# Routing between MLP and experts: order of TensorE's products, the expert list, loads and fetches at the transition

## The reference

```python
def _moe2_ref(x, w_gate, w1, w2):          # x 3072 x 512, 8 experts, w1 512 x 1024, w2 1024 x 512
    logits = x @ w_gate
    expert_idx = np.argmax(logits, axis=1)
    logits_shift = logits - logits.max(-1, keepdims=True)
    probs = np.exp(logits_shift)
    probs /= probs.sum(-1, keepdims=True) + 1e-09
    gate_w = probs[np.arange(N), expert_idx]
    for e in range(E):
        mask = expert_idx == e
        xe = x[mask]
        h = np.maximum(xe @ w1[e], 0.0)
        ye = h @ w2[e]
        out[mask] = gate_w[mask, None] * ye
```

## Time and profile before

| | us |
|---|---|
| median of 3 runs (lowest, highest) | 1026.34 (1026.3, 1027.01) |
| profiled execution | 1028.64 |
| its span | 1027.0 |
| PE busy | 999.0 (97%) |
| PEld busy | 818.5 (80%) |
| DVE busy | 647.8 (63%) |
| ACT busy | 583.8 (57%) |
| POOL busy | 403.4 (39%) |

### The profile page before, as it was taken

The page is one execution under the profiler, slowest core; times in us unless marked ns, Lnnn a source line. Parts: engine busy times, 40 slices in busy tenths (PEclk is TensorE's granted clock), DMA queues, the critical chain, the costliest instruction groups (busy, mean ns, idle before and its releaser), DMA issues.

```text
span 1027.0 us, 19832 instructions
## 1 busy us (share of the span) xinstructions
PE 999.0 (97%) x6222; PEld 818.5 (80%) x6223; DVE 647.8 (63%) x1211; ACT 583.8 (57%) x1255; POOL 403.4 (39%) x393
## 2 busy tenths in 40 slices
PE   7988999999999999999999999998999999999998
PEld 5766778888888888888888888886788888888886
DVE  5877788878876886787778788855224424225221
ACT  7877778766776676677666776724124324225221
POOL 3676354444544554455445546621111111112111
PEclk9999999999999999999999999989999999999999
DMA  8999613940890194059001202119112412411111
GB/s 308 347 410 353 261 42 114 363 140 12 273 347 28 62 359 153 4 188 300 0 10 41 103 21 73 42 44 350 69 41 67 174 50 83 152 41 41 32 51 36
DMA packets 58272, 143.26 MB, mean 139 GB/s; under 512 B 4711, under 2 KB 10471, under 8 KB 58224
## 3 DMA queue, kind: packets, MB, share of 16 engines
q1 hardware_dynamic: 51424, 121.07, 33.3%
q0 software_dynamic: 6800, 21.56, 6.2%
HBM read 71.08 MB, written 72.32 MB: 140 GB/s over the span
## 4 chain that ended last, share of the span: by engine, by line
PE 88%; ACT 3%; DMA 3%; DVE 2%; issue 2%; SPq 1%; POOL 0%; POOLq 0%; ACTq 0%; DVEq 0%
PE PS L667 25%; PE PS L509 25%; PE PS L540 14%; PE PS L549 14%; ACT prob L815 2%; PE PS L533 2%; PE PS L687 2%; PE PS L611 1%; PE PS L526 1%; DVE PS L997 1%; DMA out<-y_sb,idx_s 1%; DMA qk<-qk_all 1%; PE PS L707 1%; PE PS L581 1%; DMA pad_rows<-rows_by_expert 1%
## 5 line engine op out<-in xcount | busy, mean ns | idle before, releaser
L509 PE MATMUL PS<-xs,weights 128*128 (+1 forms) x1152 | 282.7, 394 | 0.0
L509 PEld LDWEIGHTS PS<-xs,weights 128*128 128x128 f32 x1152 | 212.7, 188 | 43.1
L667 PE MATMUL PS<-weights,g_hi 128*128 128x512 f32 x768 | 238.0, 391 | 1.3 <-POOL g_lo L1342 0.8
L1342 POOL TENSOR_TENSOR g_lo<-g_sb,g_hi 128x512 fp32r<-128x512 f32 x96 | 124.3, 1295 | 275.2 <-ACT g_hi L895 275.2
L667 PEld LDWEIGHTS PS<-weights,g_hi 128*128 128x128 f32 x768 | 143.0, 188 | 35.0 <-issue 2.9
L667 PE MATMUL PS<-weights,g_lo 128*128 128x512 f32 x384 | 149.6, 390 | 0.0
L876 ACT ACTIVATE b_ln<-PS,cf 128x512 f32<-128x512 f32 x96 | 66.0, 687 | 141.6 <-PE PS L509 141.6
L540 PE MATMUL PS<-weights,xg_hi 128*128 (+1 forms) x448 | 143.0, 401 | 0.5 <-issue 0.5
L549 PE MATMUL PS<-weights,h_hi 128*128 (+1 forms) x432 | 135.8, 395 | 1.3 <-issue 1.3
L1345 POOL TENSOR_TENSOR den<-den,b_r 128x512 f32<-128x512 f32 x96 | 128.9, 1343 | 2.1 <-ACT b_r L903 2.1
L1046 DVE TENSOR_TENSOR xg_lo<-PS,xg_hi 128x512 fp32r<-128x512 f32 x29 | 20.0, 690 | 127.3 <-ACT xg_hi L840 127.3
(11 more groups left out here) (189 smaller groups left out, 1584.7 us busy)
## 6 DMA issues: line engine op xcount, KB each, us to landing
rows_by_expert<-pad_rows SPq DMA_DIRECT2D x16, 1799.0 KB, 20.4
e_raw<-w_exp SPq DMA_DIRECT2D x34, 512.0 KB, 6.5
qk<-qk_all SPq DMA_DIRECT2D x32, 480.0 KB, 7.0
rows_by_expert<-pad_rows SPq DMA_DIRECT2D x8, 1542.0 KB, 20.0
vw<-v_all SPq DMA_DIRECT2D x32, 384.0 KB, 6.7
rows_by_expert<-pad_rows SPq DMA_DIRECT2D x8, 1285.0 KB, 17.7
w_raw<-w_mlp SPq DMA_DIRECT2D x16, 512.0 KB, 8.5
pad_rows<-rows_by_expert POOLq DMA_DIRECT2D x30, 257.0 KB, 3.0
```

The costliest lines, as they stand in the source:

```text
L509: last = pe.matmul(PS[:, H_BANK + f % 2, :], w[:, wp], rhs, start=k == 0, stop=k == 3 * KT - 1)
L667: last = pe.matmul(PS[:, ACC_BANK + s, :], gp[:, f % 2, s * P:(s + 1) * P], w[:, wp], start=f == 0 and k == 0, stop=f == FT - 1 and k == 2)
L1342: pool.tensor_tensor(g_lo[:, q], g_sb[:], g_hi[:, q].bitcast(F32), ALU.subtract).then_inc(g_lo_done, 1)
```

## The change

- TensorE: the four transposes and four groups of logits of the last block are no longer in one piece. The first slice (`kt` 0) of tile 1's first product stands behind two of the transposes, the second between the logits, the third behind them, the fourth behind the ranks. The last part of tile 1's second product (`ft` 7) stands behind the first product of tile 2, and the signal `w2e_done` with it.
- DVE: the same 28 schedule instructions in another order: the list of experts (`sched[R_EXP]`) comes out in the middle and sets a new semaphore `list_ready`. The register load of the first expert stands ahead of the gate instructions, instead of behind the copy of the counts. Tile 1's `lower_h` waits for `sched_ready` and a register load; the second expert's splits are spread between `finish` and `lower_x`.
- ACT: `sched_ready` and its register load ahead of `upper_h(1)`; the splits spread in the same way.
- SP: the second expert's load waits for `list_ready`; the wait for the landing of tile 2 stands ahead of chunk 4; the number of experts is read behind chunk 7.
- GpSimd: the meta copy of tile 1 and the indices of tile 0 are made before the last rows are scattered. The fetch of tile t+3 stands ahead of the wait for the landing of the scatter of tile t for the first tiles, and column registers are loaded ahead of waits. In the loop the order is as before.

```diff
@@ SP
             sp.wait_ge(h_ready, STEPS)
-            sp.wait_ge(gathered, 48)
-            sp.wait_ge(sched_ready, 1)
-            experts = load_sched(sp, R_CNT, 1, 1, E)
+            sp.wait_ge(list_ready, 1)
             e = load_sched(sp, R_EXP, 1, 0, E - 1)
             for c in range(WCH):
+                if c == KT:
+                    sp.wait_ge(gathered, 48)
                 if c == WCH - 2:
                     sp.wait_ge(w2e_done, upto(w2e_done, 2))
                 sp.dma_start(e_chunk(c), w_exp[bass.ds(e, 1), c].rearrange("o p n -> (o p) n")).then_inc(eraw_in[c], 16)
+            sp.wait_ge(sched_ready, 1)
+            experts = load_sched(sp, R_CNT, 1, 1, E)
@@ TensorE
-            for s in LAST_ORDER:
+            def transpose_last(s):
...
-            for s in LAST_ORDER:
+            def logits_last(s):
...
-            last.then_inc(last_logits, 1)
-            half_product(0, 0, (0, 1))
+            transpose_last(0)
+            transpose_last(2)
+            half_product(0, 0, (0,))
+            transpose_last(1)
+            transpose_last(3)
+            logits_last(0)
+            logits_last(2)
+            half_product(0, 0, (1,))
+            logits_last(1)
+            logits_last(3).then_inc(last_logits, 1)
+            half_product(0, 0, (2,))
...
-            half_product(0, 0, (2, 3))
+            half_product(0, 0, (3,))
             half_product(0, 1).then_inc(w1e_done, 1)
...
             transpose_x(2)
-            second_product(1, 0, range(5, EKT)).then_inc(w2e_done, 1)
+            second_product(1, 0, range(5, 7))
 
             pe.wait_ge(sched_ready, 1)
             tiles = load_sched(pe, R_CNT, 0, NSUB, NSUB + E - 1)
             first_product(2)
+            second_product(1, 0, range(7, EKT)).then_inc(w2e_done, 1)
             transpose_x(3)
@@ ACT
             relu(1)
-            upper_h(1)
-            upper_x(2)
-
             act.wait_ge(sched_ready, 1)
             tiles = load_sched(act, R_CNT, 0, NSUB, NSUB + E - 1)
-            split_expert(1, range(0, 5))
+            upper_h(1)
+            split_expert(1, range(0, 3))
+            upper_x(2)
+            split_expert(1, range(3, 6))
             relu(2)
             upper_x(3)
-            split_expert(1, range(5, WCH))
+            split_expert(1, range(6, WCH))
@@ DVE
             dve.tensor_tensor(all_hot[:], desc, each(1), ALU.is_equal).then_inc(last_hot, 1)
+            first = load_sched(dve, R_CNT, 2, 0, E - 1)
...
-            first = load_sched(dve, R_CNT, 2, 0, E - 1)
             chain.need(n)
...
+            dve.tensor_tensor(sched[:, R_EXP, 0:E], twice[:, 0], twice[:, 1], ALU.add).then_inc(list_ready, 1)
...
+            dve.tensor_tensor(sched[:, R_SPLIT], row[:, 3], order[:, 1:], ALU.mult).then_inc(sched_ready, 1)
+
+            dve.wait_ge(sched_ready, 1)
+            tiles = load_sched(dve, R_CNT, 0, NSUB, NSUB + E - 1)
             lower_h(1)
+            split_expert(1, range(0, 1))
             finish(0)
+            split_expert(1, range(1, 3))
             lower_x(2)
-            tiles = load_sched(dve, R_CNT, 0, NSUB, NSUB + E - 1)
+            split_expert(1, range(3, 6))
             finish(1)
-            split_expert(1, range(0, 5))
             lower_x(3)
-            split_expert(1, range(5, WCH))
+            split_expert(1, range(6, WCH))
@@ GpSimd: fetch() is now keep_meta(t - 1) and load_tile(t, col); send_y() is split into copy_idx, send_y, land_y
-            pool.wait_ge(last_rows, 1)
-            for s in range(SUBS):
-                send_rows(s)
+            keep_meta(1)
+            copy_idx(0)
+            pool.wait_ge(last_rows, 1)
+            for s in range(SUBS):
+                send_rows(s)
             pool.wait_ge(sched_ready, 1)
+            col = col_of(2)
             pool.wait_ge(rows_sent, upto(rows_sent, 64 * BLOCKS))
-            fetch(2, col_of(2))
+            load_tile(2, col)
             send_y(0)
-            fetch(3, col_of(3))
+            col = col_of(3)
+            fetch(3, col)
+            land_y(0)
+            copy_idx(1)
             send_y(1)
-            fetch(4, col_of(4))
+            col = col_of(4)
+            fetch(4, col)
             pool.drain()
+            land_y(1)
```

More of the change, by code:

```diff
@@ L729, in _ @@
                                      stop=kt == KT - 1, skip_group_check=True)
-            last.then_inc(last_logits, 1)
-            half_product(0, 0, (0, 1))
+                return last
+            transpose_last(0)
[9 more added lines that the diff above has]
+            half_product(0, 0, (2,))
             pe.wait_ge(seen_done, upto(seen_done, NSUB - SUBS))
@@ L1214, in _ @@
             chain(dve.tensor_copy(cnt, twice[:].rearrange("p a e -> p (a e)")[:, bass.ds(first, E)]))
+            chain.ran(dve.memset(one8, 1.0))
+            n_some = chain.ran(dve.tensor_scalar(some, cnt, 0.0, None, ALU.is_gt))
             n_gt = chain.ran(dve.tensor_tensor(gt[:], cnt.unsqueeze(2).to_broadcast([P, E, SLOTS]),
                                                cst[:, C_J:C_J + SLOTS].unsqueeze(1).to_broadcast([P, E, SLOTS]), ALU.is_gt))
-            chain.ran(dve.memset(one8, 1.0))
@@ L1219, in _ @@
-            n = chain.ran(dve.tensor_scalar(some, cnt, 0.0, None, ALU.is_gt))
+            chain.need(n_some)
+            n_ocum = chain.ran(dve.tensor_tensor_scan(ocum, one8, some, 0.0, ALU.mult, ALU.add))
             chain.need(n_gt)
             n_fill = chain.ran(dve.tensor_reduce(fill, gt[:], AX.X, ALU.add))
-            chain.need(n)
-            n_ocum = chain.ran(dve.tensor_tensor_scan(ocum, one8, some, 0.0, ALU.mult, ALU.add))
+            chain.need(n_ocum)
+            n_list = chain.ran(dve.tensor_tensor(ge[:, 2, 0:E], t_row[:, 0:E].unsqueeze(2).to_broadcast([P, E, E]),
+                                                 ocum.unsqueeze(1).to_broadcast([P, E, E]), ALU.is_ge))
@@ L1224, in _ @@
             chain.need(n_fill)
             n_cum = chain.ran(dve.tensor_tensor_scan(cum, one8, fill, 0.0, ALU.mult, ALU.add))
-            n_leap = chain.ran(dve.tensor_tensor(jwrap, leap[:], fill, ALU.subtract))
-            chain.need(n_cum)
-            n = chain.ran(dve.tensor_tensor(ge[:, 0], over_t, over_e(cum), ALU.is_ge))
+            chain.need(n_list)
+            n_list = chain.ran(dve.tensor_reduce(jlist, ge[:, 2, 0:E], AX.X, ALU.add))
+            chain.ran(dve.tensor_tensor(jwrap, leap[:], fill, ALU.subtract))
@@ new lines, in _ @@
+            chain.need(n_list)
+            n_list = chain.ran(dve.tensor_scalar(twice[:, 0], jlist, float(E - 1), first_e[:, 0:1], ALU.min, ALU.add))
+            n_ge = chain.ran(dve.tensor_tensor(ge[:, 0], over_t, over_e(cum), ALU.is_ge))
+            chain.need(n_list)
+            n_list = chain.ran(dve.tensor_scalar(twice[:, 1], twice[:, 0], float(E), -float(E), ALU.is_ge, ALU.mult))
+            chain.need(n_ge)
+            n_col = chain.ran(dve.tensor_tensor(ge[:, 1], ge[:, 0], over_e(jwrap), ALU.mult))
@@ L1230, in _ @@
+            chain.need(n_list)
+            dve.tensor_tensor(sched[:, R_EXP, 0:E], twice[:, 0], twice[:, 1], ALU.add).then_inc(list_ready, 1)
+            n_ord = chain.ran(dve.tensor_tensor(ge[:, 2], ge[:, 0], over_e(some), ALU.mult))
             chain.ran(dve.memset(order[:, 0:1], 0.0))
-            chain.need(n)
-            n_col = chain.ran(dve.tensor_tensor(ge[:, 1], ge[:, 0], over_e(jwrap), ALU.mult))
-            n_ord = chain.ran(dve.tensor_tensor(ge[:, 2], ge[:, 0], over_e(some), ALU.mult))
@@ L1242, in _ @@
             n_ord = chain.ran(dve.tensor_scalar(order[:, 1:], row[:, 1], 1.0, ocum[:, E - 1:E], ALU.add, ALU.min))
-            n_list = chain.ran(dve.tensor_tensor(ge[:, 1, 0:E], t_row[:, 0:E].unsqueeze(2).to_broadcast([P, E, E]),
-                                                 ocum.unsqueeze(1).to_broadcast([P, E, E]), ALU.is_ge))
+            chain.ran(dve.tensor_copy(sched[:, R_CNT, 0:1], cum[:, E - 1:E]))
             chain.need(n_ord)
+            off = row[:, 4].bitcast(I32)
+            n_off = chain.ran(dve.tensor_scalar(off, order[:, 1:], -1.0, None, ALU.add))
@@ L1246, in _ @@
+            n_new = chain.ran(dve.tensor_tensor(row[:, 2], order[:, 1:], order[:, 0:TMAX], ALU.is_gt))
             chain.ran(dve.tensor_copy(sched[:, R_ORD], order[:, 1:]))
-            n_off = chain.ran(dve.tensor_scalar(sched[:, R_EXP], order[:, 1:], -1.0, None, ALU.add))
-            n_new = chain.ran(dve.tensor_tensor(row[:, 2], order[:, 1:], order[:, 0:TMAX], ALU.is_gt))
             chain.need(n_off)
-            n_off = chain.ran(dve.tensor_scalar(sched[:, R_OFF], sched[:, R_EXP], 1, 3, ALU.bitwise_and, ALU.logical_shift_left))
@@ L1319, in fetch @@
                 pool.dma_start(xg[:, 0:XW], tiles_dram[bass.ds(col, 1)].rearrange("o p n -> (o p) n")).then_inc(gathered, 16)
+            def fetch(t, col):
+                if due(t):
+                    keep_meta(t - 1)
+                load_tile(t, col)
             for u in range(UNITS):
@@ L1391, in _ @@
```

(2 more changed lines are left out.)

18 lines of the change are left out of this document (10 added, 8 removed).

## The result

The changed kernel took 1031.37 us (median of 7, 1027.4 to 1034.66), the kernel before 1026.83 (7 runs); ratio 1.005, 95% interval 1.0028 to 1.0071. It is slower, by 3 to 7 us. The forecast was 1023.9. Repeated beside other kernels it gave 1.0043 (1.0022 to 1.0064). The profiled execution took 1030.89, span 1029.2.

What follows compares the result with a forecast made beforehand. It took the start of tile 2's second product (720.74 us) as the bound: 3.0 us earlier, less 0.6 for half clock, gives 2.4 us and a median of 1023.9 us. Range 1019.0 to 1026.4, the forecast's own 1022.8 to 1025.0.

Steps and rivals of the forecast that it cites:

- Bound and place: The end moves only with the start of tile 2's second product, 720.74 us; afterwards TensorE is busy at full clock.
- Products between the logits: TensorE at the last logits: full clock kept, tile 1's first product ends at 684.8 instead of 686.97, gain 2.2 us.
- Schedule and list: DVE's routing: places 0.6 us later, schedule 0.2 earlier (688.3), expert list at 685.9, first early load at 686.7.
- The price of it: Last row scatter beside four early loads: 5.25 us (3.0 to 6.7), landing at 693.0; tile 2's rows at 696.7.
- ACT and DVE cost nothing: Moved halves and splits before tile 2's first product cost nothing if its rows land at 696.7; otherwise splits hold until 697.5.
- Fetches ahead of scatters: GpSimd: tile 1's scatter landing, 6.7 us, leaves the chain; tile 4's fetch at w + 4.1 takes 6.7; start 3.0 earlier.
- The new hole: TensorE before tile 2's second product: 0.7 us of work between 712.4 and 717.7, a hole of some 5 us.
- Clock in the new hole: Half clock after the hole before tile 2's second product costs 0.6 us, bounds 0 and 1.7.
- Sum: Whole kernel: 3.0 − 0.6 = 2.4 us gained, median 1023.9 us.
- the slower one: Rival, chance 0.07: early loads delay tile 2's rows past 699.8; 1028.8 to 1030.5 us.
- Light disturbance: Rival, chance 0.27: transfers barely disturb each other, tile 4's fetch takes 3.7 us; 1018.6, range 1017 to 1021.8.

Runs made afterwards that it cites:

- logits_in_one: Changed kernel with the last block's transposes and logits in one piece, two product slices behind them, two behind the ranks: 1030.78 us, 1.0028 to the kernel before.
- after_again: The changed kernel unedited, measured again on the same chip as other kernels: 1031.49 us, ratio 1.0043 to the kernel before.
- third_late: Changed kernel with one edit: the third expert's loads wait until tile 4's rows have landed. 1025.33 us, ratio 0.9978 to the kernel before.
- late_all_third: Changed kernel with second expert's loads and splits behind tile 2's rows, third expert's loads behind tile 4's: 1023.67 us, ratio 0.9960 to the kernel before.
- late_all: Changed kernel with second expert's loads behind tile 2's landing and their splits behind the split of tile 2's rows: 1028.28 us, 1.0002 to the kernel before.
- only_fetch_order: Kernel before with only GpSimd's part of the change: 1025.83 us, ratio 0.9976 to the kernel before.
- before_third_late: Kernel before with one added wait: the third expert's loads wait for the landing of tile 4's rows. 1027.21 us, ratio 0.9995.

## Why the prediction was wrong

- *Bound and place:* right. The loop is unchanged (301.3 us behind the transposes of tile 3, 300.7 before), and the transition sets the difference.
- *Products between the logits:* the place right, the gain wrong. The logits ended 7.5 us behind the start of the transposes of tile 0, 7.8 forecast. "I take full clock" failed: half clock came at 680.6, behind the ranks, and covered six of the 512-column matmuls where it had covered twelve. The first product of tile 1 ended 14.34 us behind the transposes of tile 0 instead of 15.31, a gain of 1.0 and not 2.2, and even this is luck. In the four other profiles with the logits in one piece it ended at 13.7 (granted clock 0.88 from the transposes to there, 0.78 in the profile before); in the nine with products between them at 13.8 to 14.5 (0.88) six times and at 15.3 to 15.5 (0.78) three times. No gain is shown, and logits_in_one bears that out. In the changed kernel this part lay under the wait for rows.
- *Schedule and list:* right. The first load went out at 685.93; 686.7 less the 0.5 by which this execution is ahead is 686.2.
- *The price of it* is the step that failed first. "I take 693.0 (5.25, as the four loads are nearly through)", "6.7 at most". It took 8.34, and 7.29 to 7.99 in the three other profiles with early loads and this order (after_again, third_late, logits_in_one), beyond the upper bound that I had from the nearest rows. The bound came from a scatter and fetches that met the loads at other moments. Here the scatter was issued 1.0 us behind the first of the four loads and landed when they were through: 2.09 MB of loads and 0.76 MB of scatters passed in 686 to 696, and it landed at 695.3. Most of the rest follows: rows at 698.93 instead of 696.7, a wait of 3.60 instead of 2, first product 30.6 us behind the transposes of tile 0 where 27.1 was forecast (27.6 before). Of these 3.5 us, 2.8 are the scatter and 0.7 the issue time ahead of the first product (701.02), which the sum had left out.
- *ACT and DVE cost nothing:* right, but only with early loads. "Without that cover the splits hold the first product until 697.5" missed the other side: without early loads they held it until 703.88. The new place of the splits was a dependency on the early loads that I had not costed.
- *Fetches ahead of scatters:* right, and the useful part: 3.35 us of T alone, 4.5 to 4.8 in late_all_third. From the end w of tile 1's second product (708.15) the fetch of tile 4 went out 3.6 us later (4.1 forecast) and took 6.85 (6.7). No wait for tile 3's rows or the relu, as forecast.
- *The new hole:* with its waits of 2.19 and 1.45 the second product of tile 2 starts 49.6 us behind the transposes of tile 0, 0.5 over before, where 3.0 under it was forecast. All of the 3.5 between is w, which came 3.7 later than forecast.
- *Clock in the new hole:* the second term that was mis-sized, 0.6 taken, 1.6 measured: the second product of tile 2 took 7.19 us to the next transposes against 5.57 before, nearly the upper bound of 1.7. In the repeat it was 7.74, 2.2 more than before and over the bound, and the second product started where it had before (49.06 us behind the transposes of tile 0, 49.08).
- *Sum:* +0.5 + 1.6 = 2.1, the measured T. Against the forecast of −2.4 that is 4.5 us, 3.5 by the later rows of tile 2 and 1.0 by the clock.
- *Rivals:* the slower one was the mechanism, given 0.07. It needed rows later than 699.8 and they came at 698.93, which is 699.5 in the times of the profile before, 0.3 short of its point. The issue time of 0.7 that the sum had left out, and the clock's 1.6, made the loss all the same. "The four loads are over by 694" was true within a us and no argument: the scatter landed with them. The profiled execution is 2.25 us over before, under this rival's 2.5 to 4; the median of 1031.37 is above its range. Light disturbance was wrong.

  The Trainium skill (DMA: Bandwidth & Descriptors, "Queues, rings and completion order") has the engines take turns between queues packet by packet, from which the prediction estimated 3.7 us for a transfer of this size. The trace does not agree: the scatter took 8.34.

Shown by taking away, in T: early loads and splits +3.8, the third expert's loads over the fetch of tile 4 +4.8 (+4.3 in late_all), the fetch order −3.4 to −4.8. So the change carried one good part and one that cost as much. The third expert's loads are not part of it: they lay over the fetch of tile 4 before as well (7.23 us), where holding them back moved nothing. What the parts leave over, late_all against only_fetch_order, is 1.7 us of loss.

Not settled: the medians lie 4.5 us apart in the first comparison and 3.2 in the second, the profiled spans 2.2 and 2.0. The changed kernel's executions spread over 7 us (spans 1025.7 to 1033.0), the shortest with the highest mean clock (0.998), the longest with the two lowest (0.990, 0.991), which fits further half clock in those executions; no profile of one was taken, so this is not shown. Nor was the move of tile 1's last part behind the first product of tile 2 tried alone; it is in every kernel derived from the changed one. The fetch order together with the third expert's late loads, on the kernel before, was not run either, and it is the smallest version that might be as fast as late_all_third.

## What to carry to other kernels

A load that nobody needs soon is not free because the queue is idle when it starts: ask which short transfer on the path will be in flight with it. Here such a scatter, 3.0 us alone, landed when the loads were through, and that is the price to put in as the upper bound. Start bulk loads on the landing of the last transfer that matters, and move what consumes them to the same place, or an engine in order will sit before data that is late on purpose. When a good edit and a bad one come together, the edit alone on the kernel before and the kernel after without it tell them apart; one of the two is not enough (before_third_late alone would have said that the third expert's loads do not matter). And before a gain of 1 or 2 us of half clock goes into a sum, look at more than one execution: here its price differed by up to 1.6 us between profiles of the same order.

## What the runs showed that I had not expected

- A 257 KB scatter issued 1 us behind the first of four 512 KB loads took 7.29 to 8.34 us in four profiles. Scatters of about that size (tile 1's y) beside eight loads took 6.70 to 7.6, and last row scatters without loads 3.0 to 4.9. Half as many loads beside it did not make it quicker.
- The fetch of tile 4 took 2.9 to 3.5 us in the five profiles read where the third expert's loads were held back, and 6.1 to 7.4 in the eight with them.
- After the logits half clock was moved, not removed: in the changed kernel it starts behind the ranks, at 680.6, where the kernel before had it from the end of the logits at 678.1 on. How long it lasts differed between profiles of one order, as said above.
